# Row sums' reciprocals: one small transpose and six transfers in place of six transposes and copies

## The chip, the cores and the metric

One core of a Trainium2 chip runs the whole program. The metric is the device time of one execution in microseconds; lower is better. Engines are named as the profile names them: PE (matmuls and transposes), DVE, ACT and POOL (elementwise work), SP (issues the transfers). Each engine executes its own list in order and waits at semaphores.

## The reference

Attention over 4 x 8 heads of 576 rows and head size 64, with a decay and a causal mask, and then two MLP layers over the 2304 rows:

```python
scores = scale * q @ k.T + (cum[:, None] - cum[None, :])    # cum = cumsum(log f); causal mask
attn = exp(scores - max(scores))
attn = attn / (sum(attn) + 1e-9)                            # the reciprocals of this case
x = attn @ v                                                # 2304 x 512 over all heads
h = x @ moe_w_in;  x = relu(h) ** 2 @ moe_w_out
h = x @ moe2_w_in; out = smooth(h) @ moe2_w_out             # 0, (h+1)^2/4 or h by range
```

All in float32; the kernel splits each operand into a high and a low part and multiplies three times.

## The kernel before

The attention works on 16 pairs of heads (g). The scores of a pair lie in nine tiles of 128 rows: tile 0 holds the last 64 rows of both heads, and the tiles 1 to 8 hold the row blocks 3, 3, 2, 2, 1, 1, 0, 0 of head 0 and head 1 by turns. The product with V is computed transposed: the 128 partitions are the head sizes of both heads (64 + 64), and the 576 columns are the rows of the attention. The sum of a row stands on the row's own partition, so its reciprocal has to get from a column of `rinv` (128 x 9) into `rbc` (128 x 576), where partition p holds the reciprocals of all 576 rows of p's head.

Each step s of the attention runs the lists `PE_ORDER`, `ACT_ORDER` and `DVE_ORDER`, written out by hand in the file. An item is (what, number, back): back 0 is pair s, back 1 the pair before. The step after the last pair runs `PE_LAST`, `ACT_LAST` and `DVE_LAST`, in which the first four blocks of the MLP (U on PE, G on ACT and DVE, weight splits W) fill the place of the next pair's scores. The items:

- S: scores of a group of tiles on PE; maximum of one tile on DVE; exponential and sum of one tile on ACT.
- T: transposes of a piece of the exponentials on PE into one of the two banks 4 and 5; its high part on ACT (L666), its low part on DVE (L847). `bank_free` makes a T or R on PE wait until the item that had the same bank before it has been read. The banks go by turns along the T and R items of the list.
- O: ten products with V on PE; O7 and O8 end the large output, O9 is the small one (rows 0 to 127).
- R on DVE: adds 1e-9 to the nine sums and takes the reciprocals (L872, L874).
- V on ACT (`spread_r`, L672): repeats 8 of the 9 reciprocal columns 64 times each into `rexp`, 128 x 512.
- R on PE (`turn_r`): R0 makes four transposes of 128 x 128 of `rexp` (L1092); R1 makes two of the ninth column (L1097, L1098). R on ACT (`put_r`) copies both into `rbc` (L681, L683).
- M on DVE (`put_x`): M0 (L882) and M1 (L887, two instructions) multiply the outputs by `rbc` into x. After M1 a semaphore (x_put) lets O0 of the next pair overwrite the output bank.

POOL splits q, k and v of the pairs to come and masks the decay (L555). SP loads them: `reload(par, g)` waits until POOL has split the q and k of pair g-2, issues the load of q and k, waits until DVE has all maxima of pair g-2, issues four transfers of decay rows (L426, L431; each repeats one row of DRAM over 64 or 128 partitions), waits for POOL's split of v, and issues the load of v. The weights of the MLP come in 256 KB transfers (L453, L456) through the same queue. Their slots lie over the buffers of the attention, so slots from 4 on wait until these are free.

Of the kernel before, what the change touches and what calls it, by code (L numbers as in the profile page):

```python
# [5 lines left out]
F32 = mybir.dt.float32  # L6
# [4 lines left out]
P = 128  # L11
# [5 lines left out]
def mixed_attention_mlp(nc, qk, v, f, w_in1, w_out1, w_in2, w_out2, scratch, out):  # L17
    PAIRS = qk.shape[0]
# [40 lines left out]
    def queries(h0, h1, j, at_col=0):  # L59
# [14 lines left out]
    LAST_PIECE = [0, 1, 1, 2, 2, 3, 4, 5, 6, 6]  # L74
    NR = 2


    PE_ORDER = [("S", 0, 0), ("T", 2, 1), ("S", 1, 0), ("S", 2, 0), ("T", 3, 1), ("O", 0, 1),
# [3 lines left out]
    ACT_ORDER = [("S", 7, 1), ("T", 3, 1), ("S", 8, 1), ("T", 4, 1), ("S", 0, 0), ("T", 5, 1),  # L82
                 ("T", 6, 1), ("V", 0, 1), ("T", 0, 0), ("S", 1, 0), ("S", 2, 0), ("R", 0, 1),
                 ("R", 1, 1), ("S", 3, 0), ("S", 4, 0), ("S", 5, 0), ("T", 1, 0), ("T", 2, 0),
                 ("S", 6, 0)]
    DVE_ORDER = [("S", 0, 0), ("T", 1, 1), ("T", 2, 1), ("S", 1, 0), ("T", 3, 1), ("R", 0, 1),
                 ("T", 4, 1), ("S", 2, 0), ("T", 5, 1), ("S", 3, 0), ("S", 4, 0), ("T", 6, 1),
                 ("T", 0, 0), ("S", 5, 0), ("S", 6, 0), ("S", 7, 0), ("S", 8, 0), ("M", 0, 1),
                 ("M", 1, 1)]

    PE_LAST = [("U", 0, 1), ("T", 2, 1), ("T", 3, 1), ("U", 1, 1), ("T", 4, 1), ("O", 0, 1),
# [3 lines left out]
    ACT_LAST = [("T", 3, 1), ("W", 4, 1), ("S", 7, 1), ("S", 8, 1), ("T", 4, 1), ("T", 5, 1),  # L97
                ("G", 0, 1), ("V", 0, 1), ("T", 6, 1), ("G", 1, 1), ("R", 0, 1), ("R", 1, 1),
                ("W", 5, 1), ("G", 2, 1), ("G", 3, 1)]
    DVE_LAST = [("T", 1, 1), ("T", 2, 1), ("T", 3, 1), ("R", 0, 1), ("T", 4, 1), ("W", 4, 1),  # L100
                ("G", 0, 1), ("T", 5, 1), ("T", 6, 1), ("G", 1, 1), ("M", 0, 1), ("G", 2, 1),
                ("G", 3, 1), ("W", 5, 1), ("M", 1, 1)]
    assert RUN[0] == 0
# [31 lines left out]
    with ctx:  # L135
# [3 lines left out]
        def sem(name):  # L139
            return ctx.enter_context(nc.semaphore(name))  # L140
# [50 lines left out]
        rbc = at("rbc", [P, S], F32, 1)  # L191
        rexp = at("rexp", [P, 2 * QB, DH], F32, 1)
        nmax = at("nmax", [P, 2, NT], F32, 1)
# [149 lines left out]
        rinv_done = sem("rinv_done")  # L343
        rexp_done = sem("rexp_done")
        r_turned = sem("r_turned")
        r_put = sem("r_put")
        p_turned = sem("p_turned")
        p_hi = sem("p_hi")
# [63 lines left out]
        def _(sp):  # L412
# [57 lines left out]
            load_v(1, 1)  # L470
            def reload(par, g):

                sp.wait_ge(qk_ready, g - 1)
                load_qk(par, g)
                sp.wait_ge(max_ready, NT * (g - 1))
                load_cb(par, g)
                sp.wait_ge(v_ready, g - 1)
                load_v(par, g)

            with sp.Fori(0, (PAIRS - 10) // 2) as m:  # L480
                for par in range(2):
                    reload(par, 2 * m + 2 + par)
            for g in range(PAIRS - 8, PAIRS):
                reload(g % 2, g)
                if g in (PAIRS - 8, PAIRS - 5, PAIRS - 3, PAIRS - 2):
                    load_w((PAIRS - 8, PAIRS - 5, PAIRS - 3, PAIRS - 2).index(g))

            for n in range(FREE, 2 * FT):
                load_w(n)
# [159 lines left out]
        def _(act):  # L649
# [18 lines left out]

            def spread_r(par, g):

                act.wait_ge(rinv_done, g + 1)
                nc.scalar.activation(rexp[:, :, :], rinv[:, par, 1:NT].unsqueeze(2).broadcast_to([P, NT - 1, DH]), copy)\  # L672
                    .then_inc(rexp_done, 1)

            def put_r(par, g, n):

                act.wait_ge(r_turned, NR * g + n + 1)
                if n == 0:
                    act.wait_ge(x_put, g + 1)
                if n == 0:  # L680
                    last = nc.scalar.activation(rbc[:, 0:QB * P], banks[:, ring_bank("R", n, par), 0:QB * P], copy)  # L681
                else:
                    last = nc.scalar.activation(rbc[:, QB * P:S], banks[:, ring_bank("R", n, par), TAIL:P], copy)  # L683
                last.then_inc(r_put, 1)

# [51 lines left out]
            def do(what, n, g, par, m2, m, dt, s):  # L737
                if what == "S":
                    exp_tile(par, g, n)
                if what == "T":  # L740
                    hi_p(par, g, n)
                if what == "R":
                    put_r(par, g, n)
                if what == "V":
                    spread_r(par, g)
# [72 lines left out]
        def _(dve):  # L818
# [196 lines left out]
        def _(pe):  # L1015
# [4 lines left out]
            def bank_free(what, n, s):  # L1020
# [64 lines left out]
            def turn_r(par, g, n):  # L1085

                ps = banks[:, ring_bank("R", n, par), :]
                if n == 0:
                    pe.wait_ge(rexp_done, g + 1)
                    for i in range(QB):  # L1090
                        u = TILES.index((0, i)) - 1
                        last = turn(ps[:, i * P:(i + 1) * P],  # L1092
                                    rexp[:, u:u + 2, :].rearrange("p h d -> p (h d)"), ident[:, :])
                else:

                    pe.wait_ge(rinv_done, g + 1)
                    turn(ps[:, 0:P], rinv[:, par, 0:1].broadcast_to([P, P]), ident[:, :])  # L1097
                    last = turn(ps[0:64, TAIL:TAIL + P], rinv[:, par, 0:1].broadcast_to([P, 64]), ident[:, :])  # L1098
                last.then_inc(r_turned, 1)

# [39 lines left out]
            def up(layer, c, j):  # L1140
# [154 lines left out]
```

## Time and profile before

| | us |
|---|---|
| median of 3 runs | 991.56 (991.34 to 991.62) |
| the profiled execution, own time | 991.63 |
| its span, first to last instruction | 989.8 |
| attention: 16 steps and the start | up to about 189 |
| last step of the attention with the first MLP blocks | about 189 to 205 |
| rest of the MLP, PE 100% busy | about 205 to 989.8 |

A busy time is the sum of the records of an engine without overlap. A matmul's record includes its latency, so the distance between two starts is what it holds PE for. An idle time is told with the engine and line that ended it.

### The profile page before, as it was taken

How to read it: one execution, taken by the hardware profiler on the slowest of the kernel's cores; microseconds unless marked ns; L12 is line 12 of the kernel's file. 1: busy time of each engine (PE TensorE's matmuls, PEld its weight loads, DVE VectorE, ACT ScalarE, POOL GpSimd, SP SyncE). 2: the span in 40 equal slices, each digit the busy share in tenths (PEclk: the TensorE clock that was granted, in tenths of full speed). 3: DMA queues.
4: the chain of work that ended last, by engine and by line, in shares of the span. 5: the costliest groups of instructions: out<-in, count | busy, mean ns of one | idle time of the engine just before them, and what ended most of it. 6: DMA issues, size and time to landing. Idle time of an engine off the chain costs nothing.

```text
span 989.8 us, 14986 instructions
## 1 busy us (share of the span) xinstructions
PE 983.0 (99%) x5266; PEld 859.0 (87%) x5266; DVE 516.8 (52%) x1079; ACT 405.3 (41%) x888; POOL 153.0 (15%) x208
## 2 busy tenths in 40 slices
PE   8999999999999999999999999999999999999998
PEld 7888888999988888888889998988888888888997
DVE  7888888765422332232233566555455445544544
ACT  7888888854322232232223454232222223223322
POOL 7877888600000000000000000000000000000000
PEclk9999999999999999999999999999999999999999
DMA  6445555232000000000002440000001000000100
GB/s 220 147 145 177 158 175 195 65 121 72 1 1 1 1 0 0 0 0 1 1 1 64 127 129 22 1 32 1 1 1 43 0 0 33 10 1 1 43 1 32
DMA packets 39473, 50.01 MB, mean 51 GB/s; under 512 B 2656, under 2 KB 26720, under 8 KB 39424
## 3 DMA queue, kind: packets, MB, share of 16 engines
q1 hardware_dynamic: 39424, 49.37, 15.6%
q8 instruction: 30, 0.49, 0.2%
q14 instruction: 19, 0.16, 0.1%
HBM read 44.56 MB, written 4.79 MB: 50 GB/s over the span
## 4 chain that ended last, share of the span: by engine, by line
PE 96%; DVE 2%; ACT 1%; issue 0%; DMA 0%
PE banks L1167 39%; PE banks L1198 19%; PE banks L1184 19%; PE banks L1121 7%; PE banks L1066 5%; PE banks L1076 5%; PE banks L1092 1%; PE banks L1125 1%; PE banks L1117 0%; ACT W L689 0%; DMA fs<-f_dram 0%; DVE W L894 0%; DVE r L928 0%; DVE r L922 0%; ACT r L716 0%
## 5 line engine op out<-in xcount | busy, mean ns | idle before, releaser
L1167 PE MATMUL banks<-xs,W 128*128 128x512 f32 (+1 forms) x1728 | 383.7, 371 | 0.0
L1167 PEld LDWEIGHTS banks<-xs,W 128*128 128x128 f32 x1728 | 317.9, 188 | 47.4
L1198 PE MATMUL banks<-W,gs 128*128 128x512 f32 x864 | 209.1, 390 | 0.2 <-DVE gs L905 0.2
L1184 PE MATMUL banks<-gs,W 128*128 128x512 f32 (+1 forms) x960 | 209.0, 367 | 0.0
L1184 PEld LDWEIGHTS banks<-gs,W 128*128 128x128 f32 x960 | 175.1, 188 | 22.5
L1198 PEld LDWEIGHTS banks<-W,gs 128*128 128x128 f32 x864 | 161.7, 188 | 32.9 <-DVE gs L905 0.5
L905 DVE TENSOR_TENSOR gs<-r,gs 128x512 fp32r<-128x512 f32 (+1 forms) x160 | 102.3, 639 | 113.0 <-ACT gs L710 62.1
L716 ACT ACTIVATE r<-r 128x512 f32<-128x512 f32 (+1 forms) x80 | 47.2, 590 | 217.2 <-DVE r L924 217.2
L912 DVE TENSOR_TENSOR r<-r 128x512 f32<-128x512 f32 (+1 forms) x80 | 51.0, 638 | 160.9 <-ACT r L707 160.9
L707 ACT ACTIVATE r<-banks 128x512 f32<-128x512 f32 (+1 forms) x80 | 44.3, 554 | 177.3 <-PE banks L1167 176.5
L922 DVE TENSOR_SCALAR r<-banks 128x512 f32<-128x512 f32 (+1 forms) x80 | 50.9, 636 | 76.0 <-PE banks L1167 75.7
L1121 PE MATMUL banks<-pT,vs 128*128 128x448 f32 (+2 forms) x384 | 86.9, 348 | 0.0
L660 ACT ACTIVATE pr<-pr,nmax 128x576 f32<-128x576 f32 (+2 forms) x144 | 82.7, 581 | 0.6 <-DVE nmax L862 0.6
L928 DVE TENSOR_TENSOR r<-banks,r 128x512 f32<-128x512 f32 (+1 forms) x80 | 51.1, 639 | 50.2 <-ACT r L716 50.0
L710 ACT ACTIVATE gs<-r 128x512 fp32r<-128x512 f32 (+1 forms) x80 | 47.2, 590 | 70.3 <-DVE r L912 53.8
L847 DVE TENSOR_TENSOR pT<-banks,pT 128x256 fp32r<-128x256 f32 (+1 forms) x144 | 70.0, 515 | 7.7 <-ACT pT L666 5.9
L666 ACT ACTIVATE pT<-banks 128x256 fp32r<-128x256 f32 (+1 forms) x144 | 61.5, 459 | 25.7 <-PE banks L1076 24.0
L719 ACT ACTIVATE gs<-r 128x512 fp32r<-128x512 f32 (+1 forms) x80 | 47.2, 589 | 57.0 <-DVE r L928 55.3
L1076 PE MATMUL banks<-ident,pr 128*128 128x128 f32 x384 | 60.9, 274 | 0.2 <-ACT pr L660 0.2
L1121 PEld LDWEIGHTS banks<-pT,vs 128*128 128x128 f32 x384 | 57.6, 190 | 0.9
L1066 PE MATMUL banks<-qk 128*128 128x288 f32 (+4 forms) x480 | 56.9, 328 | 0.0
L1066 PEld LDWEIGHTS banks<-qk 64*128 64x128 f32 (+1 forms) x480 | 42.8, 186 | 10.6 <-issue 6.8
(87 smaller groups left out, 692.7 us busy)
## 6 DMA issues: line engine op xcount, KB each, us to landing
qk_raw<-qk_dram SPq DMA_DIRECT2D x15, 608.0 KB, 6.2
W_raw<-moe_w_in_dram SPq DMA_DIRECT2D x32, 256.0 KB, 2.8
W_raw<-moe_w_out_dram SPq DMA_DIRECT2D x32, 256.0 KB, 3.0
cb<-cum_scratch SPq DMA_DIRECT2D x30, 256.0 KB, 4.4
v_raw<-v_dram SPq DMA_DIRECT2D x16, 320.0 KB, 5.3
cbt<-cum_scratch SPq DMA_DIRECT2D x30, 144.0 KB, 3.0
out_dram<-x SPq DMA_DIRECT2D x3, 1024.0 KB, 4.2
out_dram<-x SPq DMA_DIRECT2D x1, 768.0 KB, 3.5
```

Of the source, the lines that this page charges most:

```text
L660: nc.scalar.activation(t, t, ACT.Exp, bias=nmax[:, par, u:u + 1], scale=-1.0, accum_out=rsum[:, par, u:u + 1]).then_inc(exp_done, 1)
L666: last = nc.scalar.activation(in_pT(part, 0), in_bank(part, n, par), copy)
L847: last = V.tensor_tensor(in_pT(part, 1), in_bank(part, n, par), in_pT(part, 0).bitcast(F32), ALU.subtract)
L905: V.tensor_tensor(gs[:, j % GR, 1, 0:width(c)], r[:, j % RR, 0:width(c)], gs[:, j % GR, 0, 0:width(c)].bitcast(F32), ALU.subtract).then_in ...
L912: V.tensor_tensor(t, t, t, ALU.mult).then_inc(g_done, 1)
L928: V.tensor_tensor(t, h_ps(j, c), t, ALU.max).then_inc(g_done, 1)
L1066: last = mm(score_ps(u, WIDTH[u])[:, n0:n1], qk2[rows, par, a, i * P:(i + 1) * P], qk2[rows, par, b, QW + n0:QW + n1], start=(t == 0 and n ...
L1076: last = turn(ps[:, c:c + P], pr[:, par, OFF[u] + j * P:OFF[u] + (j + 1) * P], ident[:, :])
L1121: last = mm(out_ps[:, c:S - P], vj, pT[:, b, u + (2 if j == 0 else 0):u + LEN[j], :].rearrange("p u c -> p (u c)"), start=False, stop=(n = ...
L1167: last = mm(h_ps(j, c, layer == 0), W[:, j, a, 0, t * P:(t + 1) * P], xs_of(layer, c)[:, b, t, 0:width(c)], start=(t == 0 and a == b), sto ...
L1184: last = mm(banks[:, t, 0:width(c)], W[:, j, a, 1, t * P:(t + 1) * P], gs[:, j % GR, b, 0:width(c)], start=(j == 0 and a == b == 0), stop= ...
L1198: last = mm(banks[:, t, :], gs[:, j % GR, a, t * P:(t + 1) * P], W[:, j, b, 1, :], start=(j == 0 and a == b == 0), stop=(j == FT - 1 and a ...
```

## The change

1. ACT's V item, `rexp`, the six transposes and the two copies go. R on PE is now one transpose of `rinv` (128 x 9) into nine rows of a bank. R on ACT copies these 9 x 128 values into a new tile `rT`, whose row u holds the reciprocals of tile u.
2. SP issues six transfers inside the SBUF for each pair (`spread_r`): four that write 128 x 128 of `rbc` each, from two rows of `rT` repeated 64 times each, and two that write 64 x 64 each from a half of row 0.
3. M0 on DVE waits for these six transfers (rbc_in, 6 x 16) in place of ACT's copies. SP's `reload(par, g)` issues the six of pair g-3 between its load of q and k and its wait for the maxima. Those of the last pairs follow behind the loop, between the loads of weights: the slots 4 to 6 are loaded ahead of the last pair's six, the rest behind them.
4. All six lists of items are new. The T and R items are now eight in a step, nine before.

```diff
-    NR = 2
+    SPREADS = QB + 2
-    PE_ORDER = [("S", 0, 0), ("T", 2, 1), ("S", 1, 0), ("S", 2, 0), ("T", 3, 1), ("O", 0, 1),
-                ("O", 1, 1), ("T", 4, 1), ("O", 2, 1), ("O", 3, 1), ("T", 5, 1), ("O", 4, 1),
-                ("O", 5, 1), ("T", 6, 1), ("O", 6, 1), ("T", 0, 0), ("O", 7, 1), ("S", 3, 0),
-                ("S", 4, 0), ("R", 0, 1), ("R", 1, 1), ("O", 8, 1), ("O", 9, 1), ("T", 1, 0)]
+    PE_ORDER = [("S", 0, 0), ("S", 1, 0), ("T", 3, 1), ("O", 0, 1), ("T", 4, 1), ("O", 1, 1),
+                ("O", 2, 1), ("O", 3, 1), ("T", 5, 1), ("O", 4, 1), ("T", 6, 1), ("O", 5, 1),
+                ("O", 6, 1), ("R", 0, 1), ("S", 2, 0), ("S", 3, 0), ("T", 0, 0), ("O", 7, 1),
+                ("O", 8, 1), ("S", 4, 0), ("O", 9, 1), ("T", 1, 0), ("T", 2, 0)]
...
+    ACT_ORDER = [("T", 2, 1), ("S", 6, 1), ("S", 7, 1), ("S", 8, 1), ("T", 3, 1), ("T", 4, 1),
+                 ("S", 0, 0), ("T", 5, 1), ("T", 6, 1), ("R", 0, 1), ("S", 1, 0), ("S", 2, 0),
+                 ("S", 3, 0), ("T", 0, 0), ("S", 4, 0), ("S", 5, 0), ("T", 1, 0)]
+    DVE_ORDER = [("S", 0, 0), ("T", 3, 1), ("T", 4, 1), ("R", 0, 1), ("S", 1, 0), ("T", 5, 1),
+                 ("S", 2, 0), ("T", 6, 1), ("S", 3, 0), ("S", 4, 0), ("S", 5, 0), ("S", 6, 0),
+                 ("T", 0, 0), ("S", 7, 0), ("S", 8, 0), ("M", 0, 1), ("M", 1, 1), ("T", 1, 0),
+                 ("T", 2, 0)]
...
+    PE_LAST = [("U", 0, 1), ("T", 3, 1), ("O", 0, 1), ("O", 1, 1), ("T", 4, 1), ("O", 2, 1),
+               ("O", 3, 1), ("O", 4, 1), ("T", 5, 1), ("O", 5, 1), ("U", 1, 1), ("T", 6, 1),
+               ("U", 2, 1), ("O", 6, 1), ("R", 0, 1), ("O", 7, 1), ("U", 3, 1), ("O", 8, 1),
+               ("O", 9, 1)]
...
+            def spread_r(g):
+                sp.wait_ge(r_put, g + 1)
+                for i in range(QB):
+                    u = TILES.index((0, i))
+                    sp.dma_start(rbc[:, i * P:(i + 1) * P],
+                                 rT[u:u + 2, :].unsqueeze(1).broadcast_to([2, 64, P])).then_inc(rbc_in, 16)
+                for h in range(2):
+                    sp.dma_start(rbc[64 * h:64 * h + 64, QB * P:S],
+                                 rT[0:1, 64 * h:64 * h + 64].unsqueeze(1).broadcast_to([1, 64, TAIL]))...
...
+            def reload(par, g, spread=None):
                 sp.wait_ge(qk_ready, g - 1)
                 load_qk(par, g)
+                if spread is not None:
+                    spread_r(spread)
                 sp.wait_ge(max_ready, NT * (g - 1))
                 load_cb(par, g)
...
             def put_r(par, g, n):
+                act.wait_ge(r_turned, g + 1)
+                act.wait_ge(x_put, g + 1)
+                nc.scalar.activation(rT[0:NT, :], banks[0:NT, ring_bank("R", n, par), 0:P], copy).then_inc(r_put, 1)
...
             def put_x(g, n, b, dt):
-                    dve.wait_ge(r_put, NR * (g + 1))
+                    dve.wait_ge(rbc_in, 16 * SPREADS * (g + 1))
...
             def turn_r(par, g, n):
+                pe.wait_ge(rinv_done, g + 1)
+                turn(ps[0:NT, 0:P], rinv[:, par, :], ident[:, :]).then_inc(r_turned, 1)
```

## Rows read from the trace of the kernel before

**Rows 1.** Page, part 1 and part 4: busy time by engine; last chain by engine.

```profile
span 989.8 us, 14986 instructions
...
PE 983.0 (99%) x5266; PEld 859.0 (87%) x5266; DVE 516.8 (52%) x1079; ACT 405.3 (41%) x888; POOL 153.0 (15%) x208
...
PE 96%; DVE 2%; ACT 1%; issue 0%; DMA 0%
```

**Rows 2.** Engines busy in one attention step: length, busy by engine, clock, DMA.

```profile
core 0: us, PE busy (x) PEld busy (x) DVE busy (x) ACT busy (x) POOL busy (x), PEclk, DMA share, GB/s
131.09:142.66 11.57, 11.57 (x94) 10.27 (x93) 9.96 (x32) 9.95 (x31) 9.74 (x14) 1.00 0.49 153
```

**Rows 3.** PE in time order, same step: start, length, line, shapes, count.

```profile
134.34 0.55 PE L1076 MATMUL banks<-ident,pr 128*128 128x128 f32 x3
134.64 0.50 PE L1117 MATMUL banks<-pT,vs 128*128 128x64 f32 x3
...
139.01 0.27 PE L1081 MATMUL banks<-ident,pr 128*128 128x128 f32 x1
...
140.99 0.66 PE L1092 MATMUL banks<-ident,rexp 128*128 128x128 f32 x4
141.48 0.27 PE L1097 MATMUL banks<-ident,rinv 128*128 128x128 f32 x1
141.59 0.27 PE L1098 MATMUL banks<-ident,rinv 128*64 128x128 f32 x1
141.62 0.85 PE L1121 MATMUL banks<-pT,vs 128*128 128x448 f32 x3
```

**Rows 4.** PE's costliest group of reciprocal transposes, whole span.

```profile
L1092 PE MATMUL banks<-ident,rexp 128*128 128x128 f32 x64 | 10.4, 286 | 0.0
```

**Rows 5.** ACT groups: busy, mean ns, idle before.

```profile
L666 ACT ACTIVATE pT<-banks 128x256 fp32r<-128x256 f32 x48 | 16.5, 379 | 1.5 <-PE banks L1076 1.5
...
L672 ACT ACTIVATE rexp<-rinv 128x512 f32<-128x512 f32 x16 | 9.9, 621 | 0.0
L681 ACT ACTIVATE rbc<-banks 128x512 f32<-128x512 f32 x16 | 9.6, 601 | 2.1
...
L683 ACT ACTIVATE rbc<-banks 128x64 f32<-128x64 f32 x16 | 3.5, 218 | 0.2 <-PE banks L1098 0.2
```

**Rows 6.** DVE in time order: last maximum, the two products, what follows.

```profile
130.63 0.09 DVE L866 DVE_READ_ACCUMULATOR2_ANT nmax<- 128x1 f32 x1
131.18 0.62 DVE L882 TENSOR_TENSOR x<-banks,rbc 128x448 f32 x1 [0.47 <-PE banks L1121]
131.82 0.59 DVE L887 TENSOR_TENSOR x<-banks,rbc 64x128 f32 x2
...
133.46 1.35 DVE L847 TENSOR_TENSOR pT<-banks,pT 128x256 fp32r<-128x256 f32 x3
```

**Rows 7.** SP queue in time order, same step.

```profile
130.74 1.14 SPq L426 DMA_DIRECT2D cbt<-cum_scratch  x2
131.92 1.10 SPq L431 DMA_DIRECT2D cb<-cum_scratch  x2
...
133.57 0.43 SPq L416 DMA_DIRECT2D qk_raw<-qk_dram  x1
```

**Rows 8.** Page, part 6: DMA issues, size, median us to landing.

```profile
W_raw<-moe_w_in_dram SPq DMA_DIRECT2D x32, 256.0 KB, 2.8
...
cbt<-cum_scratch SPq DMA_DIRECT2D x30, 144.0 KB, 3.0
...
cum_scratch<-cum SPq DMA_DIRECT2D x1, 72.0 KB, 1.7
```

**Rows 9.** DMA of 207.5 to 216 us, two slots of weights: packets, MB, busy share.

```profile
q1 hardware_dynamic: 1344, 1.05, 38.1%
```

**Rows 10.** PE in time order at the start: 30 transposes after idle time.

```profile
1.53 5.08 PE L1134 MATMUL banks<-ident 128*128 128x128 f32 x30 [1.53 <-POOL ident L512]
```

More of the change, by code:

```diff
@@ L74, in mixed_attention_mlp @@
     LAST_PIECE = [0, 1, 1, 2, 2, 3, 4, 5, 6, 6]
-    NR = 2
-    PE_ORDER = [("S", 0, 0), ("T", 2, 1), ("S", 1, 0), ("S", 2, 0), ("T", 3, 1), ("O", 0, 1),
[3 rows of a table removed]
[L82 to L89, printed above, removed]
@@ L93, in mixed_attention_mlp @@
-    PE_LAST = [("U", 0, 1), ("T", 2, 1), ("T", 3, 1), ("U", 1, 1), ("T", 4, 1), ("O", 0, 1),
[3 rows of a table removed]
[L97 to L102, printed above, removed]
+    SPREADS = QB + 2
@@ new lines, in mixed_attention_mlp @@
+    PE_LAST = [("U", 0, 1), ("T", 3, 1), ("O", 0, 1), ("O", 1, 1), ("T", 4, 1), ("O", 2, 1),
+               ("O", 3, 1), ("O", 4, 1), ("T", 5, 1), ("O", 5, 1), ("U", 1, 1), ("T", 6, 1),
+               ("U", 2, 1), ("O", 6, 1), ("R", 0, 1), ("O", 7, 1), ("U", 3, 1), ("O", 8, 1),
+               ("O", 9, 1)]
+    ACT_LAST = [("S", 6, 1), ("S", 7, 1), ("S", 8, 1), ("T", 2, 1), ("W", 4, 1), ("T", 3, 1),
+                ("T", 4, 1), ("T", 5, 1), ("G", 0, 1), ("G", 1, 1), ("T", 6, 1), ("G", 2, 1),
+                ("R", 0, 1), ("W", 5, 1), ("G", 3, 1)]
@@ L103, in mixed_attention_mlp @@
+    DVE_LAST = [("T", 3, 1), ("R", 0, 1), ("T", 4, 1), ("T", 5, 1), ("G", 0, 1), ("G", 1, 1),
+                ("T", 6, 1), ("G", 2, 1), ("W", 4, 1), ("G", 3, 1), ("W", 5, 1), ("M", 0, 1),
+                ("M", 1, 1)]
     assert RUN[0] == 0
@@ L191, in mixed_attention_mlp @@
         rbc = at("rbc", [P, S], F32, 1)
-        rexp = at("rexp", [P, 2 * QB, DH], F32, 1)
+        rT = at("rT", [P, P], F32, 1)
         nmax = at("nmax", [P, 2, NT], F32, 1)
@@ L343, in mixed_attention_mlp @@
         rinv_done = sem("rinv_done")
-        rexp_done = sem("rexp_done")
         r_turned = sem("r_turned")
         r_put = sem("r_put")
+        rbc_in = sem("rbc_in")
         p_turned = sem("p_turned")
@@ L470, in _ @@
             load_v(1, 1)
-            def reload(par, g):
+            def spread_r(g):
[6 more added lines that the diff above has]
+                    sp.dma_start(rbc[64 * h:64 * h + 64, QB * P:S],
+                                 rT[0:1, 64 * h:64 * h + 64].unsqueeze(1).broadcast_to([1, 64, TAIL]))                        .then_inc(rbc_in, 16)
+            def reload(par, g, spread=None):
                 sp.wait_ge(qk_ready, g - 1)
                 load_qk(par, g)
+                if spread is not None:
+                    spread_r(spread)
                 sp.wait_ge(max_ready, NT * (g - 1))
@@ L478, in reload @@
                 load_v(par, g)
-            with sp.Fori(0, (PAIRS - 10) // 2) as m:
+            reload(0, 2)
+            reload(1, 3, 0)
+            with sp.Fori(1, (PAIRS - 10) // 2) as m:
                 for par in range(2):
-                    reload(par, 2 * m + 2 + par)
+                    reload(par, 2 * m + 2 + par, 2 * m + par - 1)
             for g in range(PAIRS - 8, PAIRS):
-                reload(g % 2, g)
+                reload(g % 2, g, g - 3)
                 if g in (PAIRS - 8, PAIRS - 5, PAIRS - 3, PAIRS - 2):
                     load_w((PAIRS - 8, PAIRS - 5, PAIRS - 3, PAIRS - 2).index(g))
-            for n in range(FREE, 2 * FT):
+            spread_r(PAIRS - 3)
+            spread_r(PAIRS - 2)
+            early_w = (after_qk - FREE * SLOT) // SLOT
+            for n in range(FREE, FREE + early_w):
+                load_w(n)
+            spread_r(PAIRS - 1)
+            for n in range(FREE + early_w, 2 * FT):
                 load_w(n)
@@ L667, in hi_p @@
                 last.then_inc(p_hi, 1)
[L669 to L673, printed above, removed]
             def put_r(par, g, n):
[L677 to L684, printed above, removed]
+                act.wait_ge(r_turned, g + 1)
+                act.wait_ge(x_put, g + 1)
+                nc.scalar.activation(rT[0:NT, :], banks[0:NT, ring_bank("R", n, par), 0:P], copy).then_inc(r_put, 1)
             def split_w(n):
@@ L743, in do @@
                     put_r(par, g, n)
-                if what == "V":
-                    spread_r(par, g)
                 if what == "W":
@@ L1037, in bank_free @@
                 if kind == "R":
-                    pe.wait_ge(r_put, NR * g + k + 1)
+                    pe.wait_ge(r_put, g + 1)
             def scores(par, g, n):
@@ L1087, in turn_r @@
                 ps = banks[:, ring_bank("R", n, par), :]
[L1088 to L1099, printed above, removed]
+                pe.wait_ge(rinv_done, g + 1)
+                turn(ps[0:NT, 0:P], rinv[:, par, :], ident[:, :]).then_inc(r_turned, 1)
             def product_v(par, g, n):
@@ L1150, in up @@
                     pe.wait_ge(p_lo, NP * PAIRS)
-                    pe.wait_ge(r_put, NR * PAIRS)
+                    pe.wait_ge(r_put, PAIRS)
                 elif first and j in (6, 7):
```

3 rows, old and new, of the table PE_LAST are left out of this document.

## The prediction

> **What bounds the kernel now.** I read the busy times first, then the chain that ended last: PE is busy 983.0 of 989.8 us and holds 96% of the chain [rows 1]. So a gain must take time from PE, and a loss must be an idle time that PE does not have now. Then I read one step of the attention: 11.57 us, PE busy throughout, clock 1.00, but DVE with 9.96 us, ACT with 9.95 and POOL with 9.74 close behind [rows 2]. The chain names only PE, yet DVE can wait only some 1.6 us in a step. The last view is the time order of PE, DVE and SP in that step, which gives the distances used below. The profiled execution took 991.63 us (span 989.8, 1.8 around it) and the median of the runs is 991.56, so sums against the one hold for the other.
>
> **What PE gets back.** The reciprocals' transposes hold PE from 140.99 to 141.62, 0.63 us [rows 3]. A single one of them holds it 0.11 (141.48 to 141.59), and its record is about 0.27 long, latency included [rows 3, 4]. One remains: 0.63 - 0.11 = 0.52 us for a step, 16 steps: 8.3 us. Without any new wait a step would be 11.05 us. The reorder takes out none of the other PE items. It could remove a small gap or open one; I count nothing for it, and 0.2 us a step either way as the bound.
>
> **What ACT gets back.** The spread (621 ns) and two copies (601 and 218) go; one copy of 128 columns on nine partitions comes, between the rows of 64 and 256 columns, 218 and 379 ns: I take 0.27 [rows 5]. ACT has no idle-free stretch that ends a chain, so this is worth nothing in itself. DVE's and POOL's work is unchanged.
>
> **The new chain.** What was a copy on ACT is now a chain over SP and the DMA engines. Let t = 0 be the start of R on PE.
> - The transpose 0.27, the copy 0.27, and about 0.05 for each of two semaphores: rT is ready at 0.65.
> - SP issues six transfers in a row. Its issues stand 0.43 to 0.59 us apart now (two in 1.18 us from 130.74 to 131.92, 0.43 for one of q and k) [rows 7]. So the sixth starts issuing 5 x 0.5 = 2.5 us after the first, 2.15 to 2.95.
> - A transfer needs from issue to landing 1.7 us at the least (72 KB) and 2.8 to 3.0 for those of 256 and 144 KB [rows 8].
> - The packets. No transfer in the trace before has fewer than 32 rows in its outermost dimension; the four large ones of the change read two rows, each repeated 64 times, in packets of 512 B. Bound below: they spread over 16 engines like all others, and their packets cost nothing beside the landing time. Bound above: only two engines work, one for each source row, 64 packets each, and the four transfers stand behind one another. A 512 B packet costs more than its share by bytes and less than the mean packet in a stretch of weights: 1344 packets, 1.05 MB, 38.1% of 16 engines x 8.5 us = 51.8 us of engine time [rows 9]; by bytes 25 ns, on the mean 38.5. I take 27 ns, near the byte share because a short packet is mostly bytes there too. 4 x 64 x 27 ns = 6.9 us (6.4 to 9.9).
>
> I take the upper case, two engines. The outermost dimension of the source holds two entries, and a split into sixteen would have to cut the repeated dimension inside it. With a weight transfer's 2.8 us less its 32 packets per engine (512 / 16 x 27 ns = 0.9), the fixed part is 1.9 us. So L, from R on PE to `rbc` complete, is 0.65 + 1.9 + 6.9 + 0.1 for the two small transfers = 9.6 us.
>
> The Trainium skill speaks on this point, in "DMA: Bandwidth & Descriptors", section "Why a DMA increments its semaphore by 16 and not by 1": a transfer is split along each side's slowest dimension that is not 1, over the largest number of engines up to 16 that divides both sizes, and a small number means the lowest-numbered engines. For 2 and 128 that is two engines, the same two for all four transfers. By a spread over 16 engines the sum would instead be that of the second rival below. No row here shows a transfer split so.
>
> **Who waits for it.** M0 waits for `rbc`, and DVE works in order: behind M0 stand M1, T1, T2 and all of the next step. On PE, T3 is in the way before O0 is: there are eight T and R items now, T3 and T1 fall on the same bank, and `bank_free` makes T3 wait for DVE's T1. From `rbc` complete: M0 0.64 (131.18 to 131.82), M1 0.59, T1 half of the 1.35 us that three such instructions took, 0.67 [rows 6], a semaphore 0.1: T3 starts at L + 2.0. From T3 to the end of O6, behind which R stands in the new order, PE needs the same eleven items as in the trace before from 134.34 to 139.01: 4.67 us [rows 3]. So a step can't be shorter than L + 2.0 + 4.67 = L + 6.67. It costs nothing below L = 11.05 - 6.67 = 4.4 us, and the change as a whole loses from L = 4.9 on, where this is 11.57. Before, the last maximum ended at 130.7 and M0 waited only for PE's product, until 131.18 [rows 6]: there was no such chain.
>
> With L = 9.6 a step is 16.3 us; it contains 16.3 - 11.05 = 5.2 us of idle PE. This falls between R of one pair and T3 of the same pair's successor, 15 times: 78 us. PE does T1, T2, S0 and S1 before it stops. DVE's 10 us, ACT's 9 and POOL's 9.7 fit easily in 16.3.
>
> **The other edits.** The six issues stand in SP's queue ahead of the wait for the maxima. They need at most 3.5 us of it; the last maxima of that step need S4, which stands behind S2, S3, T0, O7 and O8 on PE, some 3 us after R, and DVE's work on it, so the decay transfers leave at about their time. If two engines are still at work on `rbc`, the decay rows land up to 4 us later; POOL masks them for a pair that PE reaches a whole step later, so with a longer step this is hidden. Without that cover it would cost those 4 us once a step, but not beyond the idle time already counted. In the last step the load of slot 7 now stands behind the six transfers; R of the last pair is followed by O7 to O9, and U3 to U5 and D0, D1, over 10 us, so `rbc` at 9.6 comes about in time, but DVE, held at M0, is late with the weight split of slot 6: I count 1.5 us, between 0 and 5.
>
> **Sum.** 991.6 - 8.3 + 78 + 1.5 = 1062.8, about 1063 us. With packets at 25 ns and 38.5 ns and the landing part between 1.4 and 2.2, L is 8.6 to 12.8, the stall 4.2 to 8.4 us a step, and the time 1048 to 1111.
>
> **Rivals.**
> - *The clock falls in the idle stretches.* Now it is 1.00 in a step without any idle PE [rows 2]. The 30 transposes at the start, after idle time, took 5.08 us, 0.17 each [rows 10], against 0.11 in the step: some ran at the lower level of 1.2 GHz. If each stall of 5 us leaves PE at 1.2 GHz for half of the 4.67 us up to the next R, a step gets 2.3 us longer: 15 x 2.3 = 35, about 1098 us. For: the stalls would be as long as nothing in this trace. Against: PE works two thirds of the time.
> - *Sixteen engines, issue bound.* Then L = 0.65 + 2.5 + 2.5 = 5.6, a step 12.3, the stall 1.2 x 15 = 18 us: 991.6 - 8.3 + 18 = about 1001. For: all transfers in the trace spread so. Against: none has two rows outermost.
> - *Faster: the chain fits.* Place: between R and M0. If the transfers spread, each is issued in 0.36 us and the last lands 1.7 us later like the small store [rows 8], L = 0.65 + 1.8 + 1.7 = 4.15, under the 4.4 from which nothing waits: 991.6 - 8.3 = 983.3. It decides at L = 4.9. For: PE has 11.05 - 4.67 = 6.4 us of other items between R and T3. Against: three low ends at once.
>
> **Chances.** Forecast (two engines, clock kept) 0.50; clock falls too 0.22; sixteen engines and slower 0.12; faster 0.13; within 0.2%, which is about what a measurement of this kernel can tell from no change, 0.03. So slower has 0.84. The forecast alone spans 1048 to 1085. The range must take in the clock's case and most of the issue-bound one: 996 to 1112.
>
> **What would show it.** In the trace after: L1092 gone, one transpose per step; an idle time of PE of about 5 us before the second item of T in a step (T3), put down to DVE's T1, and one of DVE of over 5 us before M0, put down to a DMA of `rbc`; transfers of `rbc` landing some 3.8 us after issue for the first and more for each further; attention steps of 16 us. Wrong if DVE does not wait at M0, or if the four large transfers land in 2 us each: then the packets were spread. If steps are over 18 us, look at the granted clock.

## The result and the profile after

The changed kernel took 1143.31 us (1140.38 to 1145.15, 4 runs), the kernel before 991.59 (991.34 to 991.94, 4 runs) on the same chip: a ratio of 1.1524 [1.1509, 1.1538], 152 us slower. The prediction was 1063, with a range up to 1112. The direction was right, the loss twice as large as predicted, and outside the range. The profiled execution took 1140.38 us (span 1138.6), so it is at the low end of its runs.

The page of the changed kernel, its parts 1, 2, 4 and 5 cut to a few lines [rows 1 has those of before]. The PEclk line is the granted clock in 40 slices of 28 us, in tenths (9 is 90% or more).

```profile
span 1138.6 us, 14801 instructions
...
PE 1015.7 (89%) x5186; PEld 886.0 (78%) x5186; DVE 518.4 (46%) x1079; ACT 391.3 (34%) x856; POOL 153.7 (14%) x208
...
PEclk9778778888778999999999999999999999999999
...
PE 77%; SPq 9%; DMA 7%; DVE 3%; issue 2%; ACT 2%; DVEq 0%; ACTq 0%
...
L1084 PE MATMUL banks<-ident,pr 128*128 128x128 f32 x384 | 73.5, 323 | 111.9 <-DVE pT L855 111.9
```

Three things are to be seen. PE fell from 99% of the span to 89%, and 111.9 us of its idle time stand ahead of one line, the transposes T, behind DVE's T. The chain, which named only PE before, now holds 16% of SP's queue and DMA. And PE's busy time rose by 33 us although it has 80 instructions fewer: the granted clock is between 0.7 and 0.9 of full speed from the second slice to the thirteenth, almost the whole attention, that is, PE spends part of it at 1.2 GHz instead of 2.4. From slice 14 on, in the feed-forward part, it is full again.

One step, the windows view from T3 to T3 [rows 2 has that of before, 11.57 us at clock 1.00]:

```profile
core 0: us, PE busy (x) PEld busy (x) DVE busy (x) ACT busy (x) POOL busy (x), PEclk, DMA share, GB/s
186.23:206.87 20.64, 13.38 (x88) 11.74 (x88) 10.12 (x33) 9.06 (x28) 10.12 (x14) 0.83 0.34 103
```

The same step in time order, PE first; a bracket is idle time and what ended it.

```profile
186.23 0.90 PE L1084 MATMUL banks<-ident,pr 128*128 128x128 f32 x3 [7.16 <-DVE pT L855]
...
187.97 2.43 PE L1119 MATMUL banks<-pT,vs 128*128 128x192 f32 x9
...
192.81 0.27 PE L1097 MATMUL banks<-ident,rinv 128*9 128x128 f32 x1
...
197.64 1.96 PE L1074 MATMUL banks<-qk 128*128 128x288 f32 x12
206.87 0.90 PE L1084 MATMUL banks<-ident,pr 128*128 128x128 f32 x3 [7.26 <-DVE pT L855]
```

DVE around its product M0, and SP's queue, in which the length is that of the issuing:

```profile
204.72 0.62 DVE L890 TENSOR_TENSOR x<-banks,rbc 128x448 f32 x1 [7.33 <-DMA rbc<-rT]
...
205.98 1.35 DVE L855 TENSOR_TENSOR pT<-banks,pT 128x256 fp32r<-128x256 f32 x3
```

```profile
193.41 4.55 SPq L476 DMA_DIRECT2D rbc<-rT  x4
198.01 4.68 SPq L479 DMA_DIRECT2D rbc<-rT  x2
202.73 1.23 SPq L425 DMA_DIRECT2D cbt<-cum_scratch  x2
```

The chain of the prediction is there step by step: R starts on PE at 192.81, the first transfer leaves at 193.41 (0.60 later), M0 starts when `rbc` is complete at 204.72 (L = 11.9), T3 follows at 206.87 (2.15 behind M0). Before, M0 waited for PE only [rows 6]. Over all 16 steps L has a median of 12.1 us (11.5 to 12.6), and from R to R a step takes 21.35 us on the mean, 21.07 without the last (25.28), where before it took 11.70, and 11.58 without the last (13.45).

What the DMA engines moved from 193 to 206 us, in 40 slices of 0.325 us:

```profile
GB/s 0 0 0 0 0 39 44 43 44 43 32 19 19 19 19 19 20 20 14 22 43 44 43 43 44 54 39 21 27 27 25 24 28 25 142 220 227 229 187 222
...
rbc<-rT SPq DMA_DIRECT2D x4, 64.0 KB
```

From 194.6 to 204 the DMA engines carry almost only `rbc`, at 43 GB/s or at about 20, where the decay rows and loads right behind it run at 220. How many engines work on it is seen from the share of the 16 that is busy, here in 194.7 to 196.2 and in 196.7 to 198.9 (packets, MB, busy share):

```profile
q1 hardware_dynamic: 129, 0.07, 14.4%
```

```profile
q1 hardware_dynamic: 83, 0.04, 10.8%
```

That is 2.3 and 1.7 of 16 engines: about two, in the fast stretch and in the slow one. Divided by the packets it is 27 ns of engine time for each packet in the fast stretch and 46 in the slow one. The chain that ended last shows SP in the same step, one issue at a time:

```profile
193.41 0.61 SPq L476
...
194.67 0.93 SPq L476
...
195.64 2.32 SPq L476
...
200.49 4.04 DMA rbc<-rT
```

The first two issues take 0.61 and 0.57 us, the third and fourth 0.93 and 2.32, and the first small one 2.44.

### The profile page after: what moved, and what is told of

It is laid out like the page before. It is cut to its first block, busy times and chain, and to the rows that moved or that the text cites. A ratio compares the mean times of both kernels' runs of the same rounds, so it can differ in the third digit from the quotient of the medians.

```text
span 1138.6 us, 14801 instructions
## 1 busy us (share of the span) xinstructions
PE 1015.7 (89%) x5186; PEld 886.0 (78%) x5186; DVE 518.4 (46%) x1079; ACT 391.3 (34%) x856; POOL 153.7 (14%) x208
## 3 DMA queue, kind: packets, MB, share of 16 engines
q1 hardware_dynamic: 50304, 54.09, 15.8%
## 4 chain that ended last, share of the span: by engine, by line
PE 77%; SPq 9%; DMA 7%; DVE 3%; issue 2%; ACT 2%; DVEq 0%; ACTq 0%
PE banks L1165 33%; PE banks L1196 17%; PE banks L1182 16%; DMA rbc<-rT 6%; SPq L476 6%; PE banks L1119 5%; PE banks L1084 4%; SPq L479 3%; DVE pT L855 1%; PE banks L1115 1%; DVE x L895 0%; ACT W L699 0%; ACT rT L694 0%; PE banks L1074 0%; DVE W L902 0%
## 5 line engine op out<-in xcount | busy, mean ns | idle before, releaser
L1084 PE MATMUL banks<-ident,pr 128*128 128x128 f32 x384 | 73.5, 323 | 111.9 <-DVE pT L855 111.9
L1084 PEld LDWEIGHTS banks<-ident,pr 128*128 128x128 f32 x384 | 53.8, 166 | 119.4 <-issue 95.5
L1119 PE MATMUL banks<-pT,vs 128*128 128x448 f32 (+2 forms) x384 | 97.0, 400 | 0.0
L1119 PEld LDWEIGHTS banks<-pT,vs 128*128 128x128 f32 x384 | 75.1, 245 | 1.9
L890 DVE TENSOR_TENSOR x<-banks,rbc 128x448 f32 (+1 forms) x16 | 10.0, 625 | 120.8 <-DMA rbc<-rT 120.8
```

Of the source, the lines that this page charges most:

```text
L1084: last = turn(ps[:, c:c + P], pr[:, par, OFF[u] + j * P:OFF[u] + (j + 1) * P], ident[:, :])
L1119: last = mm(out_ps[:, c:S - P], vj, pT[:, b, u + (2 if j == 0 else 0):u + LEN[j], :].rearrange("p u c -> p (u c)"), start=False, stop=(n = ...
```

## The experiments

Each theory and its rival were put to a kernel of their own. L is again the time from R on PE to M0 on DVE, which is the whole new chain.

**Sixteen engines.** DVE writes each reciprocal eight times, so that `rT` has 72 rows, and a transfer reads 16 rows and repeats each 8 times. Count, bytes and order of the transfers stay.

```
-    rT[u:u + 2, :].unsqueeze(1).broadcast_to([2, 64, P])
+    rT[8 * u:8 * u + 16, :].unsqueeze(1).broadcast_to([16, 8, P])
...
-    V.reciprocal(rinv[:, par, :], rsum2[:, par, :])
+    V.reciprocal(rinv[:, par, :].rearrange('p (u k) -> p u k', k=8),
+                 rsum2[:, par, :].unsqueeze(2).broadcast_to([P, NT, 8]))
```

> The changed kernel with one thing altered: each reciprocal is written eight times by DVE (128 x 72), so the one transpose gives eight equal rows per tile and each of the four large transfers reads 16 rows repeated 8 times in place of two rows repeated 64 times. Same number of transfers, same bytes. Theory (two rows confine a transfer to two engines): data time almost vanishes, issues stand 0.4 to 0.6 us apart again, L (from R on PE to M0 on DVE) falls from 11.9 to about 5.3 us, a step from 20.7 to about 12.1, time about 1001 (995 to 1010), clock 1.00 throughout. Rival (repeating rows inside the SBUF is slow by itself, or the six issues are): L stays above 9 and the time above 1080.

Measured: 1024.4 us (1021.8 to 1025.72), ratio 1.0326 [1.0308, 1.0344]. L fell from 12.1 to 6.25, a step from 21.35 to 14.09. In time order, SP, DVE and PE of this kernel:

```profile
120.78 2.54 SPq L476 DMA_DIRECT2D rbc<-rT  x4
123.36 1.24 SPq L479 DMA_DIRECT2D rbc<-rT  x2
```

```profile
126.34 0.63 DVE L891 TENSOR_TENSOR x<-banks,rbc 128x448 f32 x1 [1.68 <-DMA rbc<-rT]
```

```profile
113.89 0.54 PE L1085 MATMUL banks<-ident,pr 128*128 128x128 f32 x3 [1.52 <-DVE pT L855]
...
115.07 2.43 PE L1120 MATMUL banks<-pT,vs 128*128 128x192 f32 x9
...
129.42 1.35 PE L1120 MATMUL banks<-pT,vs 128*128 128x192 f32 x9
```

Two rows at the source, not the bytes, made L long, and with the busy share above that is two engines. One rival isn't separated from it: this kernel also repeats each source row 8 times and not 64. Against it stand the two small transfers, which repeat one row 64 times. One row leaves the 64 repeats as the first dimension that is larger than 1, and they aren't held to two engines: in the changed kernel's 201.2 to 202.1, where the first of them lands among the rest, 37% of the 16 engines are busy, and in the last kernel below such a transfer lands 2.3 us after its issue. But each issue costs SP 0.63 us and not 0.5, and the run came out at 1024, not at 1001. The last two lines are the same nine matmuls in successive steps, 2.43 us and 1.35: in some steps the clock fell after PE had been idle 1.5 us, in others it did not. The first ten steps are 14.6 to 14.7 us long where the granted clock is 0.88 (four of them), and 13.0 to 14.0 where it is 1.00.

**Half the copies.** Each large transfer fills partitions 0 to 63 alone.

```
-    sp.dma_start(rbc[:, i * P:(i + 1) * P], rT[u:u + 2, :].unsqueeze(1).broadcast_to([2, 64, P]))
+    sp.dma_start(rbc[0:64, i * P:(i + 1) * P], rT[u:u + 2, :].unsqueeze(1).broadcast_to([2, 32, P]))
```

> The changed kernel with each of the four large transfers writing 32 copies of its two rows in place of 64, into partitions 0 to 63 alone; the other half of rbc holds ones, so the output is not the reference's. Theory (time goes by packets on two engines, about 70 ns for each packet pair over all): the data time halves, L falls from 11.9 to about 7.5, a step from 20.7 to about 15.5, time about 1060 (1045 to 1075). Rival (a fixed price for a transfer of two rows): L 10.5 or more, 1120 or more.

Measured: 1063.88 us (1061.96 to 1068.1), ratio 1.0727 [1.0695, 1.0759], L 7.7: as expected. 128 packets less on each of the two engines take 4.4 us off L, 34 ns a packet, between the 27 and the 46 ns of the two stretches above; the prediction had 27. DVE's whole wait ahead of its 16 M0, by the groups, first of the changed kernel, then of this one, then of sixteen engines:

```profile
L890 DVE TENSOR_TENSOR x<-banks,rbc 128x448 f32 (+1 forms) x16 | 10.0, 625 | 120.8 <-DMA rbc<-rT 120.8
```

```profile
L891 DVE TENSOR_TENSOR x<-banks,rbc 128x448 f32 (+1 forms) x16 | 10.0, 625 | 52.2 <-DMA rbc<-rT 52.2
```

```profile
L891 DVE TENSOR_TENSOR x<-banks,rbc 128x448 f32 (+1 forms) x16 | 10.0, 625 | 29.0 <-DMA rbc<-rT 29.0
```

**Kept warm, first try.** 40 transposes of the identity into a free bank ahead of S0, to tell the fallen clock from the wait.

```
                 need(pe, max_ready, NT * g + BANK_READ[n])
+                if n == 0 and not start:
+                    for _ in range(40):
+                        turn(banks[:, 2, 0:P], ident[:, :], ident[:, :])
```

> The changed kernel with 40 dummy transposes of the identity on PE ahead of the first scores of each step but the first, some 4.4 us of work in the time in which PE is idle anyway. Theory (the part of the loss beyond L is the clock that falls while PE idles): the clock stays 1.00, the stretch from T3 to R goes from 6.6 back to 4.7 us, 15 times 1.9 = 28 us less, about 1115 (1105 to 1125). Rival (that stretch is longer because of waits for DVE or ACT): no gain, 1140 or more.

Measured: 1138.25 us (1135.97 to 1140.18), ratio 1.1471 [1.1452, 1.1490], mean granted clock 0.970. A miss: 40 of them filled only part of the gap, 3 us stayed idle and the clock still fell. The experiment didn't do what it was to do, and says nothing for or against.

**Kept warm, whole gap.** The same with 72.

> kept_warm with 72 dummy transposes in place of 40, 7.9 us of work, so that PE does not idle before T3 at all. Theory (the clock falls after idle time, and its fall lengthens T3 to R): clock 1.00, T3 to R 4.7 to 4.8, a step about 19.5 in place of 20.6, time about 1125 (1118 to 1132). Rival (that stretch is long because of DVE and ACT): T3 to R stays at 6.3 or more and the time at 1138 or more.

Measured: 1124.1 us (1122.78 to 1124.31), ratio 1.1327 [1.1308, 1.1346]: as expected. One step, windows and then PE:

```profile
88.69:107.95 19.26, 19.26 (x160) 17.71 (x159) 10.02 (x35) 9.06 (x28) 7.60 (x10) 1.00 0.36 108
```

```profile
93.61 8.02 PE L1063 MATMUL banks<-ident 128*128 128x128 f32 x72
101.38 1.96 PE L1077 MATMUL banks<-qk 128*128 128x288 f32 x12
103.28 0.55 PE L1087 MATMUL banks<-ident,pr 128*128 128x128 f32 x3
...
107.95 0.27 PE L1100 MATMUL banks<-ident,rinv 128*9 128x128 f32 x1
```

PE does 8 us more work a step and the kernel is 19 us faster. From T3 to R it takes 4.67 us again (103.28 to 107.95), as before the change [rows 3], against 6.58 in the changed kernel (186.23 to 192.81). L has a median of 11.9, near the 12.1 of before. So 1.9 us a step is the clock, and it is there only because PE stands still.

**No large transfers.** `rbc` is filled once with ones; the two small transfers stay. This leaves the new order and the small transpose alone.

```
-    for i in range(QB):
-        u = TILES.index((0, i))
-        sp.dma_start(rbc[:, i * P:(i + 1) * P], rT[u:u + 2, :].unsqueeze(1).broadcast_to([2, 64, P]))...
...
+    V.memset(rbc[:, :], 1.0)
```

> The changed kernel without the four large transfers: only the two of 64 x 64 are made and waited for, so most of rbc holds ones and the output is not the reference's. Theory (the loss is all in these transfers): L about 3.5 us, under the 4.4 from which nothing waits, a step 11.05 us, time about 983 (981 to 986). Rival (the new order or the small transpose costs something too): above 988.

Measured: 992.28 us (991.63 to 995.45), ratio 1.0009 [1.0000, 1.0019]. The loss of 151 us is gone with the four transfers. But the 8.3 us that PE was to get back aren't there either: without the last, a step takes 11.60 us, at the best 11.38, not 11.05, and the last takes 15.8 against 13.45 before. L is 4.6 at the median, not 3.5, yet M0 waits for a transfer in one step only. The new order costs about what the small transpose saves.

**New order, old way.** The kernel before with the orders of the change, and its spread and transposes put where R stands now.

```
-  ("O", 6, 1), ("R", 0, 1), ("S", 2, 0), ("S", 3, 0), ("T", 0, 0), ("O", 7, 1),
+  ("O", 6, 1), ("R", 0, 1), ("R", 1, 1), ("S", 2, 0), ("S", 3, 0), ("T", 0, 0), ("O", 7, 1),
```

> The kernel before with the new lists of items, but with its own six transposes, the spread and the two copies on ACT put in at the places of the new R items. No transfers of reciprocals. Theory (the new order costs and gains nothing on PE): 991.6, between 989 and 994. Rival (the order itself brings waits): over 995.

Measured: 1005.18 us (1004.01 to 1006.82), ratio 1.0141 [1.0124, 1.0158], steps of 12.2 to 13.3. A miss for the theory that the order is free. PE in one of the steps, and what the queue of weight loads (PEld), which runs ahead of the matmuls, waited for from 10 to 190 us (us in total, times, longest):

```profile
110.02 0.32 PE L1096 MATMUL banks<-ident,rinv 128*128 128x128 f32 x1 [0.55 <-DVE pT L846]
```

```profile
PEld banks L1096 <- DVE pT L846: 5.8, 14, 0.8
```

The last of the reciprocals' items falls on a bank that DVE's T still reads. PE itself is seen waiting for it in four steps, 0.16 to 0.55 us each; in the others the wait is hidden in the latency of the matmul record before and shows only in the weight load, nearly every step. That wait is in the new order with the old items; the whole cost of the order (0.84 us a step here on the mean, 12.42 against 11.58 without the last, and 0.55 without the large transfers) isn't accounted for by it alone.

**Sixteen engines, R earlier.** R goes behind O3 in the new order, to win the time that L = 6.25 is too long.

```
-  ("O", 2, 1), ("O", 3, 1), ("T", 5, 1), ("O", 4, 1), ("T", 6, 1), ("O", 5, 1), ("O", 6, 1), ("R", 0, 1),
+  ("O", 2, 1), ("O", 3, 1), ("R", 0, 1), ("T", 5, 1), ("O", 4, 1), ("T", 6, 1), ("O", 5, 1), ("O", 6, 1),
```

> sixteen_engines with R moved forward on PE from behind O6 to behind O3 (and its copy on ACT and the reciprocals on DVE with it, in the last step too), so that the chain to M0 starts some 2.5 us earlier in the step. Theory (the rest of the loss of sixteen_engines is L = 6.2 against 4.4 us, plus the clock that its idle time brings down): T3 to R is about 2.2 us, so L + 2.15 + 2.2 = 10.6 binds nothing, no idle time before T3, steps of 11.4 to 11.8 as in no_large_transfers, 988 (985 to 993). Rival (the new order's own waits at the R item's bank bind): steps of 12, 995 or more.

Measured: 1011.99 us (1008.71 to 1016.23), ratio 1.0213 [1.0176, 1.0249]. 12 us won, 36 expected: R now waits on PE for a bank that DVE's T reads, up to 1.4 us, 6.7 us in eight of the steps. Ahead of that T on DVE stand the reciprocals and their addition, which takes up to 1.5 us here (more on it below).

**Sixteen engines, old order.** The same with the orders of the kernel before, R between O3 and T5.

> The order of the kernel before, with the new way of moving the reciprocals over 16 engines (as in sixteen_engines) and R on PE between O3 and T5, where the transposes of the kernel before stood behind S4. Theory (the new order by itself costs 0.4 us a step, the small transpose gives 0.5 us): steps of 11.0 to 11.2 us, about 983 to 986, faster than the kernel before. Rival (M0 comes too late for O0, DVE has no room): steps of 11.6 or more, 991 or more.

Measured: 1001.91 us (1001.47 to 1003.38), ratio 1.0104 [1.0088, 1.0121], steps of 11.8 to 12.6. A miss by 16 us or more: PE waits 0.23 to 0.9 us for the reciprocals in every step (5.5 us in all) and up to 1.0 us at S2 for a maximum in five (2.6 us).

**The addition of 1e-9 on DVE.** Both kernels add 1e-9 to nine sums ahead of the reciprocal. This is 128x9 elements and takes 0.16 us at the least, but not always. DVE and then POOL of the kernel without large transfers:

```profile
114.67 0.79 DVE L877 TENSOR_SCALAR rsum<-rsum 128x9 f32<-128x9 f32 x1
...
126.26 1.00 DVE L877 TENSOR_SCALAR rsum<-rsum 128x9 f32<-128x9 f32 x1
```

```profile
112.62 2.81 POOL L544 TENSOR_TENSOR qk<-qk_raw,qk 128x1216 fp32r<-128x1216 f32 x1
...
124.43 2.81 POOL L544 TENSOR_TENSOR qk<-qk_raw,qk 128x1216 fp32r<-128x1216 f32 x1
```

Both times it ends within 0.03 us of POOL's instruction (115.46 and 115.43, 127.26 and 127.24). Two kernels leave it out: the one before, and the one without large transfers.

```
-    V.tensor_scalar_add(rsum2[:, par, :], rsum[:, par, :], 1e-9).then_inc(sums_done, 1)
-    dve.wait_ge(sums_done, g + 1)
-    V.reciprocal(rinv[:, par, :], rsum2[:, par, :])
+    V.reciprocal(rinv[:, par, :], rsum[:, par, :])
```

> The kernel before without the addition of 1e-9 to the sums (DVE's L872), which is the one DVE instruction whose time varies in the traces (0.16 to 1.1 us). Control for best_try. Theory (PE is the bound there): 991.6, within 0.5.

> no_large_transfers without the addition of 1e-9; the large transfers are left out as there, so the output is not the reference's. Theory (in the new order this addition stands in the time in which POOL subtracts q and k, and waits for the end of that POOL instruction, which makes R on PE and T5 late): the idle time of PE before R goes, steps 11.4 in place of 11.4 to 12.1, time 988 to 989.5. Rival (the new order's cost is elsewhere): 991.5 or more.

Measured: 991.41 us (991.28 to 991.53), ratio 0.9997 [0.9987, 1.0006], nothing (before the change R stands late on PE, which would explain it); and 990.32 (989.75 to 990.8), 0.9985 [0.9975, 0.9994], some 2 us below the 992.28 with it, less than the 3 to 4 expected. So the addition explains a fifth of what the order costs; steps of 11.39 us and more remain, 11.53 on the mean, with no idle time ahead of R. What makes them longer than 11.05 was not tried in a run, but the weight loads give a candidate. Over 10 to 190 us, first in this kernel, then in the fastest one below, with steps of 11.05 to 11.1:

```profile
PEld banks L1069 <- DVE nmax L871: 9.3, 30, 0.3
```

```profile
PEld banks L1077 <- DVE nmax L877: 4.5, 14, 0.9
```

Here the weight loads of the scores wait 0.3 us for DVE's maxima at two places of a step, again hidden behind the matmul before. The difference, 4.8 us over some 16 steps, is 0.3 us a step, about what is missing.

**Best try.** From here on the aim is a version that wins: the old order, sixteen engines, R behind O2 in free columns of a bank outside the ring (no bank to wait for), S8 ahead of T3 on ACT, no addition, and M0 waits only for the transfers that it reads.

```
+  ("T", 4, 1), ("O", 2, 1), ("R", 0, 1), ("O", 3, 1), ("T", 5, 1), ("O", 4, 1),
...
-    RING = [item for item in PE_ORDER if item[0] in "TR"]
+    RING = [item for item in PE_ORDER if item[0] == "T"]
...
+    sp.dma_start(rbc[:, 0:P], rT[8 * u:8 * u + 16, :]...).then_inc(rbc_in0, 16)
```

> The order of the kernel before, the small transpose and six transfers over 16 engines, with R on PE behind O2, in free columns of bank 7 in place of the two banks of the T items, the ACT tile 8 ahead of ACT's T3 so that the sums are ready, the reciprocal taken without the addition of 1e-9 (a sum is at least 1, so in float32 the addition changes nothing), and M0 waiting for five transfers, M1 for the sixth. Theory (PE is the bound once L = 6.2 fits and nothing waits at R): steps of 11.05 to 11.2 us, 984 (982 to 987), faster than the kernel before. Rival (no room on DVE): steps of 11.5 or more, 990 or more.

Measured: 991.01 us (988.93 to 995.08), ratio 0.9995 [0.9985, 1.0004]. The profiled execution was its slowest, 995.08. There, without the last, six steps take 11.0 to 11.1 us, one 11.4 and seven 12.1 to 13.5. SP and DVE in a long one:

```profile
90.21 0.43 SPq L416 DMA_DIRECT2D qk_raw<-qk_dram  x1
91.64 1.95 SPq L477 DMA_DIRECT2D rbc<-rT  x3
```

```profile
99.34 0.62 DVE L892 TENSOR_TENSOR x<-banks,rbc 128x448 f32 x1 [1.83 <-DMA rbc<-rT]
```

and the landing times, issues of 88 to 106 us:

```profile
qk_raw<-qk_dram SPq DMA_DIRECT2D x2, 608.0 KB, 7.7
rbc<-rT SPq DMA_DIRECT2D x7, 64.0 KB, 4.5
```

A load of q and k, 608 KB, is issued 1.4 us ahead of the row transfers, and these land 4.5 us after issue (2.4 in the next kernel).

**Best try, transfers first.** The six are issued ahead of that load.

```
-    sp.wait_ge(qk_ready, g - 1)
-    load_qk(par, g)
     if spread is not None:
         spread_r(spread)
+    sp.wait_ge(qk_ready, g - 1)
+    load_qk(par, g)
```

> best_try with the six transfers issued ahead of the load of q and k, not behind it. In best_try half of the steps take 11.05 to 11.1 us, the 0.5 less that the small transpose should give, the others 12 to 12.8: in these M0 waits up to 2.2 us for the transfers, which took 4.5 us from issue to landing and not 2.5. Theory (their packets stood behind the 608 KB of q and k on the same 16 engines): nearly all steps 11.05 to 11.4, time 985 (983 to 988), faster than the kernel before. Rival (the late transfers have another cause, as the loads of v and weights before them): 990 or more.

Measured: 985.54 us (984.54 to 985.85, 5 runs), ratio 0.9934 [0.9920, 0.9947]: faster than the kernel before by 6 us, 0.7%, and the best of all. Its page, one step by the windows, and the landing of the row transfers over the whole span:

```profile
span 984.0 us, 14812 instructions
...
PE 977.3 (99%) x5186; PEld 852.3 (87%) x5186; DVE 515.5 (52%) x1063; ACT 390.1 (40%) x856; POOL 153.2 (16%) x208
```

```profile
76.21:87.25 11.04, 11.04 (x89) 9.75 (x88) 9.90 (x32) 8.99 (x29) 8.29 (x12) 1.00 0.71 183
```

```profile
rbc<-rT SPq DMA_DIRECT2D x64, 64.0 KB, 2.4
```

This step takes the 11.05 us that the prediction gave to a step without a new wait; the mean without the last is 11.22.

## Why the prediction was right and wrong

Two terms of the sum failed and made 66 of the 78 us that it was short. The time of the four transfers was too small, above all that of their packets (27 ns each, measured 34). And the fall of the clock while PE stands still was left out of the forecast (nothing, measured 1.9 us a step). Of the smaller terms, the end of the attention was taken as 1.5 us and was 6.5.

**Two engines: right.** The step that decided the sign held. Sixteen rows in place of two halved L (12.1 to 6.25) with the same bytes, half the packets took 4.4 us off it, and 14.4% and 10.8% of 16 engines were busy. The Trainium skill's rule on the number of engines ("DMA: Bandwidth & Descriptors", section "Why a DMA increments its semaphore by 16 and not by 1") agrees with all three.

**The structure L + 2.0 + 4.67: right.** M0 to T3 is 2.15 us, T3 to R 4.67 when the clock is full. In the kernel kept warm, 11.9 + 2.15 + 4.67 = 18.7 of a step of 19.26, and there the 72 transposes are what ends last.

**The size of L: the term of the packets was too small.** Predicted 9.6 (8.6 to 12.8), measured 12.1. In the step shown, 11.9 us, the first packet moves at 194.65 and the last of the 512 large ones at 203.5 (counted in windows of the trace). So the parts are 0.6 us up to the first issue, 1.2 to the first packet, 8.9 for the packets and 1.2 up to M0. The prediction had 0.65, then 1.9 for both fixed parts together, and 6.9. So the packets are 2.0 of the 2.3 us missing here: 8.9 us for 256 on each engine is 34 ns, as the difference of two runs gives. The 27 ns chosen near the byte share is right for the fast stretches (27) and misses the slow ones (46). The row of the weights that gave the upper bound of 38.5 ns [rows 9] was the better guide. SP's issues, up to 2.4 us and not 0.5, lie within the same stretch; whether they would have ended it last with faster packets isn't known. Times 15 steps, 2.5 us at the median are 38 us of the miss.

**The clock: the wrong case was called likeliest.** "Forecast (two engines, clock kept) 0.50; clock falls too 0.22." The clock fell. The rival's reasoning held, and its size too: 2.3 us a step estimated, 1.9 measured, 28 us in 15 steps. "Against: PE works two thirds of the time" carried no weight: the changed kernel's step has a granted clock of 0.83 on the mean with PE busy 13.4 of 20.6 us, and in some steps of sixteen engines it fell behind an idle time of only 1.5 us. Had both been taken, 1063 + 38 + 28 would have been 1129.

**The reorder at nothing: wrong, and hidden in the result.** "It could remove a small gap or open one; I count nothing for it." Without the transfers the kernel is at 992.3 where 983.3 was worked out. The bound of 0.2 us a step was too narrow: 11.60 - 11.05 = 0.55. In the changed kernel itself this counts little, for PE has idle time in each step; it shows in the last step (25.3, 4.2 above the others) and it decides what the idea is worth once the transfers are mended. PE's saving of 0.52 us was right: the best version has it in its shortest steps (11.05).

**The end of the attention: mechanism right, the term of 1.5 us too small.** Predicted: DVE, held at M0, is late with the weights of slot 6. DVE and PE there:

```profile
355.13 0.62 DVE L890 TENSOR_TENSOR x<-banks,rbc 128x448 f32<-128x448 f32 x1 [5.72 <-DMA rbc<-rT]
...
358.49 1.23 DVE L902 TENSOR_TENSOR W<-W_raw,W 128x1024 fp32r<-128x1024 f32 x1 [0.39 <-ACT W L699]
```

```profile
359.86 4.18 PE L1165 MATMUL banks<-first_xs,W 128*128 128x384 f32 x12 [4.53 <-DVE W L902]
```

4.53 us idle and 4.18 us for matmuls that take 2.24 when warm: 6.5 us, 5 over the prediction. It had counted the delay of the transfers, 9.6 us, against "over 10 us" of work, a margin that 12.1 took away.

**Sum.** 38 + 28 + 2 (M0 to T3) + 5 = 73 of the 77.6 us between the 1062.8 predicted and the 1140.4 of the profiled execution. The last step's part of the order is another 2; the remaining 2 or 3 have no name.

**The signs.** L1092 gone, DVE's wait before M0 (120.8 us in 16) and PE's before T3 (111.9 in 15), each put down to what was named, all there; the idle time was 7.5 us and not 5, the steps over 18 us. The landing time of the first transfer, predicted 3.8 us, can't be read: the page has none for `rbc` in this kernel. The decay rows behind the six transfers do come late: POOL waits 121 us for them in all (79 for `cbt`, 42 for `cb`), 28 before. No wait of PE is put down to POOL's masking, as predicted.

## What to carry to other kernels

A broadcast by DMA is cheap or dear by the size of the first dimension larger than 1 in its source: with two rows of 64 repeats L was 12.1 us, with sixteen rows of 8 repeats 6.25 for the same bytes, while one row with 64 repeats landed in 2.3 us. Writing each row eight times on DVE cost 0.4 us (a reciprocal of 128x72 takes 0.60 us, of 128x9 0.22). When a change puts a wait on a TensorE that had none, add the clock to the wait, and price it from matmul rows at either level. Cost a new order of work by itself, as one would an instruction: here it ate the whole saving, and the idea paid only in the old order, with its transfers early enough and ahead of the large load in the queue.

## What the runs showed of the hardware

- *DVE's small addition ends when POOL's instruction ends.* The 128x9 addition takes 0.16 to 2.7 us (median 0.18 in the kernel before, 0.73 without large transfers), and in the cases shown it ends with POOL's running instruction on 128x1216 elements. The Trainium skill, in "SBUF — State Buffer", section "Who interferes with whom", describes a pair of SBUF ports that DVE, in its two-port modes, and GpSimd share as an exclusive lock for a whole instruction; these rows agree, though no run here took POOL's instruction away. The reciprocal behind it keeps its 0.22 us on the mean.
- *Few engines also hold the queue.* SP's first two issues of two-row transfers took 0.61 and 0.57 us, the third 0.93, the fourth 2.32, and the small ones behind them 2.3 at the median, against 0.63 for all when the large ones were spread. So it isn't the form of the transfer that is slow to issue; that SP is held by the work still outstanding is inferred from this pattern and was not tried by itself.
- *Two rates.* The two engines moved 43 to 44 GB/s for some 2 us, then 19 to 20 for 3, in the same row of transfers, and in the same way in the other steps looked at. Why the pace halves isn't known; no experiment was made on it.
- *The clock falls after short stops.* In the kernel with sixteen engines, idle times of 1.5 to 1.6 us, a step of 13 to 14.7 us apart, were followed in some steps by matmuls at half speed (2.43 us against 1.35), in others not. The longest idle time, 2.55 us, was followed by full speed (1.35), so its length alone doesn't decide.
- *A wait on PE can hide in the weight loads.* A matmul's record includes its latency, so a short wait leaves no idle time on PE. In the new order with the old items PE shows 1.7 us of waits at L1096 and PEld 5.8 us.
